# A mixture-of-experts kernel: three scatters of one batch issued together, and four routing words loaded at the head of TensorE's expert loop

## What is computed

```
# layer 1, per token i (x: 2304 x 512)
e = argmax(x[i] @ w_gate);  keep[i] = count[e] < capacity;  count[e] += 1
out[i] = softmax_top(x[i] @ w_gate) * (relu(x[i] @ w1[e]) @ w2[e])   if keep[i] else 0
# layer 2, per row, only where x @ w_skip > 0
out[i] = x[i] + gate[i] * (relu(x[i] @ w1b[e]) @ w2b[e])
```

## Time and profile before

| | |
|---|---|
| median of three runs | 680.09 us |
| the profiled execution itself | 680.36 us |
| its span, first to last instruction | 678.8 us |
| TensorE's mean granted clock | 0.992 |
| PE busy | 661.5 us, 97% of the span |
| PE's share of the chain that ended last | 92% |
| DVE / ACT / POOL busy | 369.5 / 298.8 / 206.2 us |

### The profile page before, as it was taken

One profiled execution on the slowest core, in us unless ns is written; L12 is line 12 of the kernel. 1 busy time (PEld: TensorE's weight loads), 2 busy tenths in 40 slices (PEclk: granted clock), 3 DMA queues, 4 the chain that ended last, 5 costly groups with the idle time before them and its releaser, 6 DMA issues.

```text
span 678.8 us, 17093 instructions
## 1 busy us (share of the span) xinstructions
PE 661.5 (97%) x5584; PEld 580.3 (85%) x5585; DVE 369.5 (54%) x1029; ACT 298.8 (44%) x713; POOL 206.2 (30%) x329
## 2 busy tenths in 40 slices
PE   7999999999999999999999999999999999999997
PEld 6788888788787888898899888888899899899996
DVE  3777878887888543367633367434721453411144
ACT  3777877888784122244422244113222352311233
POOL 5633436436332212322222212122122131112112
PEclk7999999999999899999999999999999999999999
DMA  8775768657532258510711148882365778711100
GB/s 169 185 193 132 199 182 216 161 128 187 130 105 76 88 126 297 189 42 24 243 63 43 47 153 305 315 316 94 121 230 176 271 282 317 261 31 48 45 18 34
DMA packets 95615, 105.89 MB, mean 156 GB/s; under 512 B 63757, under 2 KB 63757, under 8 KB 95568
## 3 DMA queue, kind: packets, MB, share of 16 engines
q1 hardware_dynamic: 84608, 81.03, 39.1%
q0 software_dynamic: 8912, 22.36, 10.2%
q10 hardware_dynamic: 2048, 1.87, 1.1%
HBM read 83.44 MB, written 28.63 MB: 165 GB/s over the span
## 4 chain that ended last, share of the span: by engine, by line
PE 92%; DMA 3%; issue 1%; DVE 1%; ACT 1%; ACTq 0%; POOL 0%; POOLq 0%; SPq 0%; DVEq 0%
PE ps L1573 33%; PE ps L1581 25%; PE ps L1468 8%; PE ps L1419 6%; PE ps L1443 5%; PE ps L1395 3%; PE ps L1475 3%; PE ps L1545 2%; PE ps L1409 2%; DMA rows<-queue 1%; PE ps L1551 1%; PE ps L1436 1%; PE ps L1559 1%; DMA queue<-pad 1%; DMA qn<-in_q 1%
## 5 line engine op out<-in xcount | busy, mean ns | idle before, releaser
L1573 PE MATMUL ps<-xT,w 128*128 128x128 f32 x1344 | 159.8, 277 | 1.2 <-issue 1.0
L1573 PEld LDWEIGHTS ps<-xT,w 128*128 128x128 f32 x1344 | 155.5, 192 | 5.1 <-issue 3.0
L1581 PE MATMUL ps<-w_hi,hT_hi 128*128 128x512 f32 x256 | 104.7, 409 | 0.5 <-DVE hT_lo L1089 0.3
L1581 PE MATMUL ps<-w_lo,hT_hi 128*128 128x512 f32 x256 | 100.3, 392 | 0.0
L1581 PE MATMUL ps<-w_hi,hT_lo 128*128 128x512 f32 x256 | 99.7, 389 | 0.0
L1300 ACT ACTIVATE hT_hi<-ps 128x512 fp32r<-128x512 f32 x64 | 37.9, 592 | 116.0 <-PE ps L1573 116.0
L1573 PE MATMUL ps<-xT,w_last 128*128 128x128 f32 x704 | 86.3, 277 | 0.3 <-issue 0.3
L1573 PEld LDWEIGHTS ps<-xT,w_last 128*128 128x128 f32 x704 | 82.3, 192 | 3.2 <-issue 2.5
L1089 DVE SCALAR_TENSOR_TENSOR hT_lo<-ps,hT_hi 128x512 fp32r<-128x512 f32 x64 | 44.2, 691 | 63.4 <-ACT hT_hi L1300 60.3
L1295 ACT ACTIVATE w_hi<-w2all 128x1024 fp32r (+1 forms) x48 | 47.0, 1046 | 62.4 <-PE ps L1581 56.5
L545 POOL DMA_INDIRECT out<-xs,idxo x32 | 37.3, 1167 | 110.2 <-DVE xs L1122 102.7
(11 more groups left out here) (198 smaller groups left out, 1028.9 us busy)
## 6 DMA issues: line engine op xcount, KB each, us to landing
w2all<-in_moe_w SPq DMA_DIRECT2D x10, 2048.0 KB, 15.2
w<-in_moe_w SPq DMA_DIRECT2D x7, 2048.0 KB, 8.9
rows<-queue POOLq DMA_DIRECT2D x36, 257.0 KB, 3.0
w2all<-in_moe_w SPq DMA_DIRECT2D x16, 512.0 KB, 4.8
w<-in_moe_w SPq DMA_DIRECT2D x12, 512.0 KB, 3.9
w_last<-in_moe_w SPq DMA_DIRECT2D x3, 2048.0 KB
qn<-in_q SPq DMA_DIRECT2D x32, 144.0 KB, 5.0
out<-pad SPq DMA_DIRECT2D x4, 1152.0 KB, 7.1
```

The source lines that it names most:

```text
L1573: last = mm(hTp[j // 4][:, j % 4, :], w1s[slot][:, c, j * P:(j + 1) * P], xT[:, c, :], start=(c == 0), stop=(c == DC - 1))
L1581: last = mm(yp, h_[:, j, :].bitcast(f32r), w_[:, j, :].bitcast(f32r), start=(j + n == 0), stop=(j == FC - 1 and n == 2))
```

## The change

In the loop over the third batch's tiles, the wait before tile 1 is dropped, that before tile 2 stays at the same count (`STEPS * (PAIRS - 2) + 3` is 59, as `+ 1 + i` was for `i` = 2), and those before tiles 3 and 4 are dropped. In TensorE's expert loop the words of the four slots are loaded at the head of each pass of `eo`; the slot loop uses the word that is there.

```
@@ GpSimd, after the last pair
             for i in range(1, NI):
-                pool.wait_ge(pv_ready, STEPS * (PAIRS - 2) + 1 + i)
+                if i == 2:
+                    pool.wait_ge(pv_ready, STEPS * (PAIRS - 2) + 3)
                 scatter_tile(B - 2, i)
@@ TensorE, expert loop
                 with pe.Fori(0, E // WSLOT) as eo:
+                    words = [pe.value_load(tabs[phase][0:1, T_N, ds(eo * WSLOT + (E + slot), 1)], min_val=32, max_val=32 * 31 + 31)
+                             for slot in range(WSLOT)]
                     for slot in range(WSLOT):
-                        both = pe.value_load(tabs[phase][0:1, T_N, ds(eo * WSLOT + (E + slot), 1)], min_val=32, max_val=32 * 31 + 31)
+                        both = words[slot]
                         n_e = both & 31
                         with pe.If(n_e > 0):
```

## The result

| | median, runs | against before |
|---|---|---|
| before | 680.56 us, 15 | |
| after | 683.08 us, 15 | 1.0035 [1.0021, 1.0049], +2.4 us (1.4 to 3.3) |

The change makes the kernel slower by 2.4 us, where 0.6 faster was forecast. The median lies 3.6 us above the forecast time of 679.5 and just outside the range, which ended at 682.9; 0.5 of the 3.6 is before itself, 680.56 here against 680.09. The profiled execution of after took 684.39 us (span 682.8), 4.0 more than that of before.

What follows compares the result with a forecast made beforehand. TensorE's array, busy 97% of the span, was taken as the bound, so only its idle time counts. Scatters -3.9 and words +3.3 sum to -0.6 against 680.36: 679.8, median 0.27 lower, so 679.5 us; range 676.8 to 682.9.

Steps and rivals of the forecast that it cites:

- stays at 210.16: Third batch's scatters: scatter 3 keeps its wait and its issue time, so scatter 5 comes at 212.72, 3.05 us earlier.
- is worth nothing: Third batch's scatters: scatter 2, now right behind scatter 1, isn't last, so issuing it earlier gains nothing.
- the term of tile 2 in phase 1: Head of phase 1's expert loop: extra words less a 1.66 us lead, plus 0.09 for a start from standstill: +0.7 us.
- the case that the forecast rests on: Whole kernel: no fall of the clock behind the new stalls; 679.5 us, own range 678.3 to 680.5, chance 0.38.
- the chain of the load: L1545: earlier last scatter brings expert 0's first rows at 218.8, so the 2.63 us wait goes, with 0.4 us of slack.
- the clock: Behind the wait at L1545: granted clock 0.50 goes away with the idle time, -1.7 us.
- Edit 1 gives the smaller part: Rival, scatters: load late or clock low in any case, so -2.2 us there and 681.2 us in all; chance 0.12.
- the pitch of the loads: Heads of the expert loop: 0.75 us a word without overlap, so three more words put 2.25 us before the first slot.
- that rival: Words overlap at the loop heads, each further load about 0.1 us: 676.2 us, or 676.8 at half the pitch; chance 0.12.
- tile 2 of phase 0: Head of phase 0's expert loop: lead of 0.3 us against 2.25 more, start 2.0 late, loss +1.75 us.
- the slower rival: New stalls at tiles 2 and 12 lower the clock, about 1.7 us each: one 681.2, chance 0.28; both 682.9, chance 0.10.
- tiles 12, 13 and 6: Expert loop: tile 12 of phase 0 with tile 13's vanished wait +0.27 us; tile 6 of phase 1 +0.55 us.

Runs made afterwards that it cites:

- edit 1: Before with the waits ahead of scatters 2, 4 and 5 of the third batch dropped, words as before; alone 678.26 us, ratio 0.9948, in its first run.
- edit 2: Before with the four slots' words loaded at the head of each expert-loop pass, scatters as before; alone 687.03 us, ratio 1.0075, in its first run.
- e4: Before with only scatter waits moved: scatter 4 waits for the scores of step 62, scatter 5 for the rows_back of pair 14; 680.29 us, 0.9981.
- f2: Before with the four words at the head in phase 1 only, scatters as before; 682.31 us, 1.0032.
- h4: Before with the four words at the head in both phases, scatters as before, run again in the fourth series; 686.28 us, 1.0081.
- f4: Before with only the words of slots 0 and 1 at the head, those of 2 and 3 in their slots; 680.60 us, 1.0010.
- f1: Before with the four words at the head in phase 0 only, scatters as before; 682.68 us, 1.0046.
- e2: Before with the four words at the head in both phases, scatters as before, first series; 687.03 us, 1.0075.
- The second series: One chip, before at 680.05 us (29 runs): words at the head by phase, fewer words at the head, and the full change again at 684.19 us.
- the fifth: Series on one more chip, before at 682.03 us (23 runs): the scatter change alone 679.54 us, the full change 684.58 us.
- k1: Before with only the scatter waits dropped, words as before, fifth series; 679.54 us, 0.9968.
- k2: The full change against before, fifth series; 684.58 us, 1.0034.
- h3: Before with the scatter waits dropped, the loop as before, plus four extra unused word loads in tile 1 of phase 0; 676.58 us, 0.9940.
- e3: Before with only scatter 5's wait dropped, so that it follows scatter 4 at once, words as before; 679.59 us, 0.9962.
- f3: The full change against before, second series; 684.19 us, 1.0057.

## Why the prediction was wrong, step by step

Three steps failed. For edit 1 the prediction held that scatter 3 "stays at 210.16" and that scatter 2 behind scatter 1 "is worth nothing"; in executions with late increments scatter 3 came 0.5 to 0.6 us later and TensorE waited 0.4 and 1.4 us that were in no term. For edit 2 the term of tile 2 in phase 1 was too small, +0.7 for +1.6. And the case that the forecast rests on, chance 0.38, had no fall of the clock behind tile 2 of phase 0, which came in three of nine traces.

Distances between landmarks take out what varies at the start. In us, from all traces that have the stretch in that form (without e4):

| stretch | old form | new form | difference | predicted |
|---|---|---|---|---|
| scatter 1 to tile 1, increments in time | 33.8 to 33.9 (before, f2, h4) | 30.1 to 30.3 (eight) | -3.7 | -3.9 |
| the same, increments late | as above | 32.05 to 32.20 (four) | -1.8 | not seen |
| phase 0, tile 1 to 4 | 43.6 to 45.4, mean 44.4 (ten, f4 among them) | 44.9 to 48.3, mean 46.5 (nine) | +2.1 | +1.75 |
| phase 0, tile 11 to 14 | mean 45.1 | 45.3 | +0.2 | +0.27 |
| phase 1, tile 1 to 3 | 26.1 to 26.2 | 27.6 to 28.1, mean 27.8 | +1.6 | +0.7 |
| phase 1, tile 3 to 8 | mean 66.3 | mean 67.0 | +0.7 | +0.55 |

In f1 and f4, whose clock did not fall behind the old wait, the old form of the first row took 32.3 and 32.6, in e2 with the long fall 35.4: where increments are in time edit 1 saves 2.2 to 5 us by execution, and where they are late as little as 0.1 (32.3 less 32.2). The trace of before was a middling one.

- **Edit 1, the chain of the load: right, and not the whole.** Issue, landing, the 0.25 us left at L1469 and the clock came as worked out, and -3.5, -3.8 and -3.7 us were measured against -3.9. What failed is that nothing else moves: where increments come late, VectorE's copies behind the close scatters wait for them, and 2 us of the gain go into the two waits at L1476. The second series, of this kind too, gives -1.4 for edit 1 (3.9 less 5.3, by medians with intervals of 1 us and more), the fifth -2.2. The rival "Edit 1 gives the smaller part" had -2.2 as its price. That k1 hit it is luck: the rival's reasons were a late load or a low clock.
- **Edit 2, the pitch of the loads: right.** 0.75 to 0.8 us a word, no overlap, so that rival fell. The Trainium skill ("DMA: Bandwidth & Descriptors", section "Latency and other measured facts") gives a load a floor of about 600 ns and says that unrolling by four amortizes it; the loads of 295 to 320 ns at the heads, the first of phase 0 about 500 and those beside SyncE's longer still, show neither the floor nor a saving by four.
- **Edit 2, tile 2 of phase 0: mechanism right, the spread missed.** The prediction took a lead of 0.3 us from one execution. The lead goes by a DMA's landing and lies up to 2 us apart between traces; single traces lie 0.5 to 3.9 above the old mean. In three of nine (f1, h4, k2) the clock fell behind it, the slower rival in part. That the mean of 2.1 is near the forecast of 1.75 is partly luck: the six traces without the fall average 45.8, or +1.3, the three with it 48.0, or +3.6.
- **Edit 2, tile 2 of phase 1: the term mis-sized, +1.6 for +0.7.** SyncE loads a word of the same table 0.8 us after TensorE's first. That load is slow in any case (1007 ns in before, where TensorE was past its only word by then). Now TensorE's second load runs beside it and takes as long, 0.7 to 1.0 us instead of 0.3. The rest is again a lead read from one trace: the sequencer reaches the loop 9.47 us after tile 1's first matmul in before, near the earliest, and up to 10.1 us after it in others, with the words at the head (after 9.86) or without them (k1 10.06).
- **Edit 2, tiles 12, 13 and 6: right** within 0.2 us.

For after's trace the terms add up: -1.86 (32.05 less 33.91), +2.41, +0.21, +1.54, +0.73, together +3.0, and +1.0 by which its first scatter came later from the span's start, where nothing was changed: the 4.0 us of the spans. Of the prediction's miss in the median, 3 us, some 1.3 to 2.2 us are edit 2 (4.6 by the table, 5.1 and 5.5 measured alone, for 3.3) and in executions with late increments about 2 us more are edit 1. How many of the 15 runs of after were of that kind isn't known; the profiled one was.

The version that beats both kernels is edit 1 alone: 0.9945 to 0.9968 of before in four series.

## What to carry to other kernels

Work put on a sequencer is free only as far as its lead reaches; read the lead from what the sequencer last waited for, and if that is a DMA, reckon with its spread and not with one trace. The same words cost nothing measurable ahead of a wait that the sequencer sits out anyway (h3), and one more word at the head cost too little to measure (f4, +0.7 us, interval -0.6 to +2.0). Price two edits of one change apart and run each alone: here a gain of 3.7 us was hidden under a loss of 5.

## What the runs showed of the hardware

- A word load of TensorE's sequencer that ran beside SyncE's second one (L406) took 697 to 995 ns in ten of ten traces, against 295 to 320 ns for most others and about 500 for the first of phase 0. SyncE's was slow (634 to 1007 ns) with or without it; what slows them both was not tried.
- TensorE's semaphore increments appeared 0.2 to 2.2 us after the end of their matmul in 8 of 20 traces, and in none of the other 12. All of them belong to matmuls that ended within 1.3 us of the start of a DMA that GpSimd issued. Where scatters stood 1.28 us apart this cost 1.8 to 2.0 us of array time (4 of 4 traces of that kind).
- The granted clock, 1.00 before, fell to 0.50, which is 1.2 GHz, behind idle times of 1.87 (e3), 2.07 (h4), 2.49 (f1) and 2.50 us (k2), and did not behind 2.12 and 2.65 at the old wait (f1, f4), 2.19 (e2), 2.48 (after) and 2.53 (f3): the length of the idle time alone does not decide it.
